# Five products of the folded gated weight as three fp32r matmuls on split operands

## The chip, the cores and the metric

The kernel runs on one core of a Trainium2 chip, in one launch. Its time is the device time of the whole program in microseconds (us), from repeated runs. The core has five engines that run side by side and wait for each other by semaphores: TensorE (PE in the profile; its weight loads are PEld), VectorE (DVE), ScalarE (ACT), GpSimd (POOL) and SyncE (SP), which here only issues DMAs. Matmul results land in PSUM, in banks of 128 x 512 fp32 values; everything else lies in SBUF.

## The reference

The program is three layers: a linear attention with a decaying state, a mixture of eight experts (one per token, with a skip test), and a gated layer. The change concerns the last one's weights only:

```python
def _attn_ref(r, k, v, w, u):            # per step t, for all batches and heads
    cur = einsum('bhd,bhe->bhde', u[None] * k[t], v[t])
    y[t] = einsum('bhd,bhde->bhe', r[t], state + cur)
    state = w[None, :, :, None] * state + einsum('bhd,bhe->bhde', k[t], v[t])

def _moe_ref(x, w_skip, w_gate, w1, w2): # N, D, E, F = 3072, 384, 8, 1024
    xc = x[x @ w_skip > 0]
    e_idx, probs = argmax(xc @ w_gate), softmax(xc @ w_gate)
    for e in range(E):
        y[mask] = gate_w[mask, None] * (maximum(xc[mask] @ w1[e], 0) @ w2[e])
    out[do_compute] = xc + y

def _moe2_ref(x, w1, w2, w3, w_out):     # w3: 1024 x 1024, w_out: 1024 x 384
    a = x @ w1
    b = x @ w2
    h = a * b @ w3
    return (h @ w_out)
```

All inputs are fp32. Since (a * b) @ w3 @ w_out is (a * b) @ (w3 @ w_out), the kernel computes the folded weight wf = w3 @ w_out (1024 x 384) once, from the weights, and the gated layer then has one matmul less.

## The kernel before, in words

The program has a block of stages and then the gated layers. In the block, each engine runs its part of the attention (`attention`), then of the routing (`routing`: which token goes to which expert, as lists of slots), then of the experts (`experts`: eight experts, one tile of up to 224 tokens each). The order on every engine is the order in which the code is written; nothing is rearranged. Engines move on independently, held only by the waits.

The fold is cut into eight chunks of 128 rows of w3, and its pieces are put between the other work by hand. For chunk i there are five steps, all methods of `Fold`:

- `load` (SP, L58 to L61) brings chunk i of w3 (512 KB) to SBUF; `load_w_out` brings w_out in two halves (768 KB each) once.
- `turn` (TensorE, L68 to L74) transposes the chunk in eight 128x128 pieces into two PSUM banks.
- `turned` (ACT, L76 to L81) copies the two banks to `w3T`, in two halves of 128x512.
- `product` (TensorE, L83 to L95) multiplies the eight slices of 128 rows with w_out into one bank, 384 columns: fp32 operands, one `matmul` call per slice, which is two instructions in the trace. It may be cut in quarters of two slices.
- `taken` (ACT, L97 to L101) copies the bank to `wf`.

`s_T`, `s_Tout`, `s_W` and `s_Wout` count these steps, and each waits for the one before by such a count. Product 0 and turns 0 and 1 stand at the end of the attention stage, turn 2 to the first half of product 5 in the routing, the second half of product 5 behind the transposes of the first expert's tokens, product 6 behind the experts and product 7 around the start of the gated layers.

Between the fold's pieces in the routing stand the routing's own matmuls: the counts (L832 to L839, into `p_count`), which wait for `s_m` from DVE and release the chain of short DVE operations behind `s_mm`; the transposes of the gate (L842 to L844); and the list matmuls (L848 to L855, into `p_list`), which wait for the one-hot tables (`s_token`, `s_near`) and release the two DVE operations that make `slot_token`. GpSimd gathers the first expert's tokens by that list (L1042), SP loads the first expert's weights w1 and w2 (1536 KB each), and ACT and DVE split w1 in a rounded part `hi` (fp32r) and the rest `lo` (`first_w1_hi`, `first_w1_lo`, L1034 and L1037).

The expert and gated layers already run with such splits: a product x y is computed as x_hi y_hi + x_hi y_lo + x_lo y_hi, three matmuls on fp32r operands (L1265, L1281, L1508, L1523).

Of the kernel before, what the change touches and what calls it, by code (L numbers as in the profile page):

```python
# [12 lines left out]
P = 128  # L13
# [20 lines left out]
LINE = 1024  # L34
# [4 lines left out]
class Fold:  # L39
# [3 lines left out]


    def __init__(self, nc, sb, sem, ident, s_ident, w3, w_out):
# [4 lines left out]
        self.w3T = [sb(f"w3T{i}", [P, self.KF, P]) for i in range(3)]  # L50
# [4 lines left out]
        self.s_T, self.s_Tout = sem("fold_T"), sem("fold_Tout")  # L55
# [58 lines left out]
def attention(nc, env, sem, r, k, v, w, u, xbuf):  # L114
# [16 lines left out]
    with ExitStack() as ctx:  # L131
# [311 lines left out]
        def _(act):  # L443
# [83 lines left out]
        def _(dve):  # L527
# [83 lines left out]
            schedule(dve, ((masks, 0), (states, -1), (bonuses, 1), (rT_out, 1), (x_out, -1), (k_decay, 2)), 2, 1, extra)  # L611
            dve.wait_ge(s_lg, 1)
# [114 lines left out]
def routing(nc, env, NT, E, NSL, CAP, ROOM, xbuf):  # L727
# [8 lines left out]
    with ExitStack() as ctx:  # L736
# [20 lines left out]
        pos = sb("pos", [P, E, NT])  # L757
        over = sb("over", [P, E, NT])
# [53 lines left out]
        def _(pool):  # L812
# [16 lines left out]
        def _(pe):  # L829
            fold.turn(pe, 2, p_T[0])  # L830
            fold.product(pe, 1, p_W[1], (0, 1, 2))
# [8 lines left out]
            fold.product(pe, 1, p_W[1], (3,))  # L840
# [7 lines left out]
            fold.product(pe, 3, p_W[1], (0, 1, 2))  # L848
# [7 lines left out]
            fold.product(pe, 3, p_W[1], (3,))  # L856
# [29 lines left out]
        def _(dve):  # L886
# [69 lines left out]
            ex.first_w1_lo(dve)  # L956
# [732 lines left out]
```

## Time and profile before

| | |
|---|---|
| median of 3 runs | 615.23 us (614.32, 615.23, 615.3) |
| profiled execution: span from first to last instruction | 612.5 us |
| TensorE busy | 595.1 us, 97% of the span, 7355 matmul instructions |
| DVE busy | 286.4 us, 47% |
| ACT busy | 228.1 us, 37% |
| GpSimd busy | 156.5 us, 26% |
| DMA | 67.80 MB, mean 111 GB/s |
| mean granted TensorE clock | 0.994 of full speed |

The page of the profile gives the span of the profiled execution and no other time of it; the median of the timed runs is 2.7 us above that span. Busy time counts an instruction from its start to its end; matmuls overlap each other, so the spacing of their starts, and not their mean duration, tells what one costs. Idle time in front of an instruction, in square brackets at the end of a timeline row, names what ended it.

### The profile page before, as it was taken

Reading aid. Unit: us, or ns where it says so; the run is one execution under the profiler, and the core shown is the slowest. Engines: PE = TensorE matmul, PEld = TensorE weight load, DVE = VectorE, ACT = ScalarE, POOL = GpSimd, SP = SyncE. Lnnn points to the kernel's source line nnn. Section 1 sums busy time; section 2 is a strip of 40 time slices with the busy share of each in tenths; the row PEclk is TensorE's granted clock in tenths of the full one; section 3 lists DMA queues with packets and bytes.
Section 4 is the critical chain, followed back from the end, with each engine's and each line's share of the span. In section 5 each row is a group of like instructions: output and inputs, shape, how many; then the busy total and the mean of one; then the engine's idle time right before and its main releaser. Section 6 shows DMA issues by size and latency. Waiting matters only on the chain.

```text
span 612.5 us, 17307 instructions
## 1 busy us (share of the span) xinstructions
PE 595.1 (97%) x7355; PEld 532.3 (87%) x7355; DVE 286.4 (47%) x459; ACT 228.1 (37%) x410; POOL 156.5 (26%) x179
## 2 busy tenths in 40 slices
PE   6699999999999999999999999999999999999997
PEld 6699999766999999999688888888898888888886
DVE  5489889283777777774121332232132133223212
ACT  3156666444665555552321222132132122213212
POOL 7568887215055544441230000000000000000000
PEclk9899999999999999999999999999999999999999
DMA  7779997596566777630400030020011001001001
GB/s 130 133 145 187 188 184 188 206 313 241 181 237 246 277 274 271 237 130 20 164 1 0 1 103 1 1 103 1 0 57 48 1 1 51 1 1 51 1 0 52
DMA packets 104258, 67.80 MB, mean 111 GB/s; under 512 B 79708, under 2 KB 98272, under 8 KB 104216
## 3 DMA queue, kind: packets, MB, share of 16 engines
q1 hardware_dynamic: 76360, 57.91, 30.8%
q10 hardware_dynamic: 25552, 4.72, 4.1%
q0 software_dynamic: 2304, 4.59, 2.3%
q8 instruction: 29, 0.48, 0.3%
q14 instruction: 13, 0.11, 0.1%
HBM read 55.92 MB, written 12.20 MB: 111 GB/s over the span
## 4 chain that ended last, share of the span: by engine, by line
PE 50%; DVE 0%; ACT 0%; issue 0%
PE gl_pab L1508 32%; PE gl_po L1523 8%; PE p_pair L1523 8%; PE gl_pab L1496 1%; PE p_pair L93 0%; DVE gl_g_lo L1590 0%; DVE gl_g_sb L1588 0%; ACT gl_g_hi L1568 0%; ACT gl_a_sb L1565 0%; DVE gl_o_sb L1601 0%
## 5 line engine op out<-in xcount | busy, mean ns | idle before, releaser
L1588 DVE TENSOR_TENSOR gl_g_sb<-gl_a_sb,gl_pab 128x512 f32<-128x512 f32 x48 | 33.0, 688 | 186.3 <-ACT gl_a_sb L1565 186.3
L1508 PE MATMUL gl_pab<-gl_xT_hi,wm_lo 128*128 128x512 f32 x288 | 112.9, 392 | 0.0
L1508 PE MATMUL gl_pab<-gl_xT_lo,wm_hi 128*128 128x512 f32 x288 | 112.8, 392 | 0.0
L1508 PE MATMUL gl_pab<-gl_xT_hi,wm_hi 128*128 128x512 f32 x288 | 112.1, 389 | 0.0
L1565 ACT ACTIVATE gl_a_sb<-gl_pab 128x512 f32<-128x512 f32 x48 | 28.8, 599 | 183.9 <-PE gl_pab L1508 183.9
L1508 PEld LDWEIGHTS gl_pab<-gl_xT_hi,wm_lo 128*128 128x128 f32 x288 | 54.0, 188 | 11.4
L1508 PEld LDWEIGHTS gl_pab<-gl_xT_hi,wm_hi 128*128 128x128 f32 x288 | 54.1, 188 | 10.6 <-DVE gl_xT_lo L1595 0.3
L1508 PEld LDWEIGHTS gl_pab<-gl_xT_lo,wm_hi 128*128 128x128 f32 x288 | 54.0, 188 | 10.5
L1265 PE MATMUL ex_ph<-ex_xT_hi,ew_w_hi 128*128 128x224 f32 x192 | 52.9, 275 | 0.0
L1265 PE MATMUL ex_ph<-ex_xT_hi,ew_w_lo 128*128 128x224 f32 x192 | 52.7, 274 | 0.0
L1265 PE MATMUL ex_ph<-ex_xT_lo,ew_w_hi 128*128 128x224 f32 x192 | 52.7, 274 | 0.0
L1590 DVE TENSOR_TENSOR gl_g_lo<-gl_g_sb,gl_g_hi 128x512 fp32r<-128x512 f32 x48 | 33.2, 692 | 33.5 <-ACT gl_g_hi L1568 33.5
L1568 ACT ACTIVATE gl_g_hi<-gl_g_sb 128x512 fp32r<-128x512 f32 x48 | 30.3, 632 | 36.2 <-DVE gl_g_sb L1588 36.2
L1281 PE MATMUL p_pair<-ew_w_hi,ex_h_hi 128*96 128x384 f32 (+1 forms) x128 | 43.4, 339 | 0.0
L1281 PE MATMUL p_pair<-ew_w_hi,ex_h_lo 128*96 128x384 f32 (+1 forms) x128 | 43.0, 336 | 0.0
L1281 PE MATMUL p_pair<-ew_w_lo,ex_h_hi 128*96 128x384 f32 (+1 forms) x128 | 43.0, 336 | 0.0
L1042 POOL DMA_INDIRECT ew_x_in<-xbuf,slot_token x16 | 22.5, 1406 | 71.3 <-DVE ex_x_new L1392 50.3
L93 PE MATMUL p_pair<-wo,w3T 128*128 128x384 f32 x112 | 38.8, 489 | 0.5 <-PEq L1652 0.4
L1265 PEld LDWEIGHTS ex_ph<-ex_xT_hi,ew_w_hi 128*128 128x128 f32 x192 | 36.8, 192 | 0.2
L1265 PEld LDWEIGHTS ex_ph<-ex_xT_lo,ew_w_hi 128*128 128x128 f32 x192 | 36.8, 192 | 0.1
L1265 PEld LDWEIGHTS ex_ph<-ex_xT_hi,ew_w_lo 128*128 128x128 f32 x192 | 36.9, 192 | 0.0
L1523 PE MATMUL gl_po<-gl_wf_hi,gl_g_hi 128*128 128x384 f32 x96 | 33.5, 349 | 0.7 <-DVE gl_g_lo L1590 0.7
(197 smaller groups left out, 1223.3 us busy)
## 6 DMA issues: line engine op xcount, KB each, us to landing
w_in<-in_moe_w SPq DMA_DIRECT2D x8, 1536.0 KB
ew_w_in<-in_moe_w SPq DMA_DIRECT2D x8, 1536.0 KB
w_in<-in_moe_w SPq DMA_DIRECT2D x14, 512.0 KB, 9.4
k_in<-in_k SPq DMA_DIRECT2D x48, 96.0 KB
v_in<-in_v ACTq DMA_DIRECT2D x48, 96.0 KB, 3.5
r_in<-in_r SPq DMA_DIRECT2D x48, 96.0 KB
w_in<-xbuf SPq DMA_DIRECT2D x12, 384.0 KB, 4.1
out<-gl_o_sb SPq DMA_DIRECT2D x12, 384.0 KB, 2.4
```

The source lines that it names most:

```text
L93: m = pe.matmul(bank[:, 0:self.DM], self.w3T[i % 3][:, g, :], self.wo[:, g, :], start=(g == 0), stop=(g == self.KF - 1), skip_group_check= ...
L1042: pool.indirect_dma_start(self.x_in[slot][0:tokens.shape[0], i, :], None, xbuf[:, :], bass.IndirectOffsetOnAxis(ap=tokens, axis=0), bounds ...
L1265: m = pe.matmul(p_h[g][:, f % 2, 0:width(t)], a[:, k, cols], b[:, k, 0:width(t)], start=(k == 0 and n == 0), stop=(k == KD - 1 and n == 2))
L1281: m = pe.matmul(p_y[i][0:n_tok, 0:DM], a[:, f, cols], b[:, f, :], start=(f == 0 and n == 0), stop=(f == KF - 1 and n == 2))
L1496: m = pe.transpose(p_ab[part][k % 2][:, i * P:(i + 1) * P], x_in[t.slot][:, i, k * P:(k + 1) * P], ident[:, :])
L1508: m = pe.matmul(p_ab[f % 2][w][:, :], a[:, w * KD + k, cols], b[t.slot][:, k, :], start=(k == 0 and n == 0), stop=(k == KD - 1 and n == 2))
L1523: m = pe.matmul(p_o[i][:, 0:DM], a[f % 2][:, cols], b[:, f, :], start=(f == 0 and n == 0), stop=(f == KF - 1 and n == 2))
L1565: act.activation(a_sb[f % 2][:, :], p_ab[f % 2][0][:, :], ACT.Copy).then_inc(s_a, 1)
L1568: act.activation(g_hi[f % 2][:, :], g_sb[f % 2][:, :], ACT.Copy).then_inc(s_ghi, 1)
L1588: dve.tensor_tensor(g_sb[f % 2][:, :], a_sb[f % 2][:, :], p_ab[f % 2][1][:, :], ALU.mult).then_inc(s_g, 1)
L1590: dve.tensor_tensor(g_lo[f % 2][:, :], g_sb[f % 2][:, :], g_hi[f % 2][:, :], ALU.subtract).then_inc(s_glo, 1)
```

## The change

Products 1 to 5 no longer run on fp32 operands. w_out is split once into `wo_hi` and `wo_lo` (ACT converts, DVE subtracts, four quarters each). The transposes of chunks 1 to 5 are converted to fp32r by ACT (`hi`, two buffers) and the rest is subtracted into `lo` (two buffers): for chunks 1, 4 and 5 by DVE straight from PSUM (`rest_dve`), for chunks 2 and 3 by GpSimd, for which ACT also makes a plain fp32 copy (`rest_pool`). Each slice is then three matmuls on fp32r operands. Products 0, 6 and 7 stay fp32. The fourth quarters of products 1 and 3, which stood behind the counts and behind the list, now stand ahead of them with the rest. `pos` and `over` share the memory of `key` and `dif`; `wo_hi` and `wo_lo` lie where the experts' `w2_hi` and `w2_lo` lie later, and ACT's first write there waits for product 5.

```diff
-
-    def __init__(self, nc, sb, sem, ident, s_ident, w3, w_out):
+    RAW = {0: 0, 2: 1, 3: 0, 6: 0, 7: 1}
+    BY_POOL = (2, 3)
+    BY_DVE = (1, 4, 5)
...
-        self.w3T = [sb(f"w3T{i}", [P, self.KF, P]) for i in range(3)]
+        self.w3T = [sb(f"w3T{i}", [P, self.KF, P]) for i in range(2)]
+        shape = [P, self.KF, P]
+        self.hi = [sb("w3T_hi0", shape, F32R), at("w3T_hi1", shape, F32R, top - 3 * 4 * FM)]
+        self.lo = [at(f"w3T_lo{i}", shape, F32R, top - (2 - i) * 4 * FM) for i in range(2)]
...
+    def out_hi(self, act, q):
+
+        rows = slice(2 * q, 2 * q + 2)
+        act.wait_ge(self.s_wo[q // 2], 16)
+        act.activation(flat(self.wo_hi[:, rows, :]), flat(self.wo[:, rows, :]), ACT.Copy).then_inc(self.s_wohi, 1)
+
+    def out_lo(self, dve, q):
+        rows = slice(2 * q, 2 * q + 2)
+        dve.wait_ge(self.s_wohi, q + 1)
+        dve.tensor_tensor(flat(self.wo_lo[:, rows, :]), flat(self.wo[:, rows, :]), flat(self.wo_hi[:, rows, :]), ALU.subtract).then_inc(self.s_wolo, 1)
+
     def turn(self, pe, i, banks):
         wait(pe, self.s_w3[i % 3], 16 * (i // 3 + 1))
         wait(pe, self.s_Tout, 2 * i)
+        if i in (4, 5):
+            wait(pe, self.s_raw, 2 * (i - 3))
+        if i in (2, 6, 7):
+            wait(pe, self.s_dlo, {2: 2, 6: 4, 7: 6}[i])
         for g in range(self.KF):
             m = pe.transpose(banks[g // 4][:, (g % 4) * P:(g % 4 + 1) * P], self.w3_in[i % 3][:, g * P:(g + 1) * P], self.ident[:, :])
         m.then_inc(self.s_T, 1)
...
     def turned(self, act, i, banks):
         wait(act, self.s_T, i + 1)
-        wait(act, self.s_W, i - 2)
+        if i in (0, 6, 7):
+            wait(act, self.s_plo, {0: 0, 6: 4, 7: 2}[i])
+            for h in range(2):
+                act.activation(self.half(self.w3T[self.RAW[i]], h), banks[h][:, :], ACT.Copy).then_inc(self.s_Tout, 1)
+            return
+        wait(act, self.s_W, i - 1 if i > 2 else 0)
         for h in range(2):
-            act.activation(flat(self.w3T[i % 3][:, 4 * h:4 * h + 4, :]), banks[h][:, :], ACT.Copy).then_inc(self.s_Tout, 1)
+            act.activation(self.half(self.hi[i % 2], h), banks[h][:, :], ACT.Copy).then_inc(self.s_Tout, 1)
+        if i in self.BY_POOL:
+            for h in range(2):
+                act.activation(self.half(self.w3T[self.RAW[i]], h), banks[h][:, :], ACT.Copy).then_inc(self.s_raw, 1)
+
+    def rest_dve(self, dve, i, banks):
+
+        for h in range(2):
+            dve.wait_ge(self.s_Tout, 2 * i + h + 1)
+            dve.tensor_tensor(self.half(self.lo[i % 2], h), banks[h][:, :], self.half(self.hi[i % 2], h), ALU.subtract).then_inc(self.s_dlo, 1)
+
+    def rest_pool(self, pool, i):
+
+        for h in range(2):
+            pool.wait_ge(self.s_raw, 2 * (i - 2) + h + 1)
+            pool.tensor_tensor(self.half(self.lo[i % 2], h), self.half(self.w3T[self.RAW[i]], h), self.half(self.hi[i % 2], h), ALU.subtract).then_inc(self.s_plo, 1)
...
         if 0 in quarters:
-            wait(pe, self.s_Tout, 2 * i + 2)
             wait(pe, self.s_Wout, i - 1)
         n = self.KF // 4
         for q in quarters:
+            h = q // 2
+            if q % 2 == 0:
+                wait(pe, self.s_Tout, 2 * i + h + 1)
+                if i in self.BY_POOL:
+                    wait(pe, self.s_plo, 2 * (i - 2) + h + 1)
+                if i in self.BY_DVE:
+                    wait(pe, self.s_dlo, 2 * self.BY_DVE.index(i) + h + 1)
+            if i == 1:
+                pe.wait_ge(self.s_wolo, q + 1)
             for g in range(q * n, (q + 1) * n):
                 if i == 0 and g % (self.KF // 2) == 0:
                     pe.wait_ge(self.s_wo[g // (self.KF // 2)], 16)
-                m = pe.matmul(bank[:, 0:self.DM], self.w3T[i % 3][:, g, :], self.wo[:, g, :],
-                              start=(g == 0), stop=(g == self.KF - 1), skip_group_check=True)
+                if i in (0, 6, 7):
+                    m = pe.matmul(bank[:, 0:self.DM], self.w3T[self.RAW[i]][:, g, :], self.wo[:, g, :],
+                                  start=(g == 0), stop=(g == self.KF - 1), skip_group_check=True)
+                    continue
+                hi, lo = self.hi[i % 2], self.lo[i % 2]
+                for n3, (a, b) in enumerate(((hi, self.wo_hi), (hi, self.wo_lo), (lo, self.wo_hi))):
+                    m = pe.matmul(bank[:, 0:self.DM], a[:, g, :], b[:, g, :],
+                                  start=(g == 0 and n3 == 0), stop=(g == self.KF - 1 and n3 == 2), skip_group_check=True)
         if 3 in quarters:
             m.then_inc(self.s_W, 1)
...
                 if f is y_out and at(c, j, NT - 1):
                     fold.turned(act, 0, [p_AU[:, i, :] for i in range(2)])
+                if f is y_out and at(c, j, NT):
+                    for q in range(3):
+                        fold.out_hi(act, q)
                 if f is y_out and at(c, j, NT + 2):
                     fold.turned(act, 1, [p_R[:, i, :] for i in range(2)])
+                    fold.out_hi(act, 3)
                     act.wait_ge(s_Y, BASE + NT + 1)
...
             schedule(dve, ((masks, 0), (states, -1), (bonuses, 1), (rT_out, 1), (x_out, -1), (k_decay, 2)), 2, 1, extra)
+            for q in range(3):
+                fold.out_lo(dve, q)
+            fold.rest_dve(dve, 1, [p_R[:, i, :] for i in range(2)])
+            fold.out_lo(dve, 3)
             dve.wait_ge(s_lg, 1)
...
+        pos, over = key, dif
...
                 pool.memset(x[:, :], 0.0).then_inc(s_clear, 1)
+            for i in fold.BY_POOL:
+                fold.rest_pool(pool, i)
...
             fold.turn(pe, 2, p_T[0])
-            fold.product(pe, 1, p_W[1], (0, 1, 2))
+            fold.product(pe, 1, p_W[1])
             pe.wait_ge(s_m, 2)
...
             pe.matmul(p_tot, tb.ones[:, :], last[1], start=False, stop=True, skip_group_check=True).then_inc(s_mm, 1)
-            fold.product(pe, 1, p_W[1], (3,))
             fold.turn(pe, 3, p_T[1])
             pe.wait_ge(s_gate, 1)
...
             fold.product(pe, 2, p_W[0])
             fold.turn(pe, 4, p_T[0])
-            fold.product(pe, 3, p_W[1], (0, 1, 2))
+            fold.product(pe, 3, p_W[1])
             pe.wait_ge(s_near, 1)
...
             m.then_inc(s_list, 1)
-            fold.product(pe, 3, p_W[1], (3,))
             fold.turn(pe, 5, p_T[1])
             fold.product(pe, 4, p_W[0], (0, 1))
...
             dve.sem_inc(env["s_listed"], 1)
-            ex.first_w1_lo(dve)
+            fold.rest_dve(dve, 4, p_T[0])
+            ex.first_w1_lo(dve, (0, 1))
+            fold.rest_dve(dve, 5, p_T[1])
+            ex.first_w1_lo(dve, (2, 3))
...
+        self.w2_hi, self.w2_lo = sb("w2_hi", [P, KF, DM], F32R), sb("w2_lo", [P, KF, DM], F32R)
...
             def w2_part(t, g):
+                if g == 0 and is_first(t):
+                    act.wait_ge(fold.s_W, 6)
                 if g == 0:
...
+        behind = nc.sbuf_base + 5 * 4 * KD * FM
+        env["fold"].wo_hi, env["fold"].wo_lo = (at(n, [P, FM // P, DM], F32R, behind + i * 4 * DM * FM // P) for i, n in enumerate(("wo_hi", "wo_lo")))
```

On TensorE, around product 1 and the counts in the routing stage, this is the order before (`w_in` are the buffers of w3's chunks, `ro_pT` the banks of the transposes, `p_pair` those of the products):

```order
L73 MATMUL ro_pT<-ident,w_in 128x128 x8
L93 MATMUL p_pair<-wo,w3T 128x384 x6
L834 MATMUL ro_p_count<-tb_mine,tb_before 128x192
...
L839 MATMUL ro_p_count<-ro_earlier,tb_ones 128x8
L93 MATMUL p_pair<-wo,w3T 128x384 x2
L73 MATMUL ro_pT<-ident,w_in 128x128 x8
```

and after the change, where of the 24 matmuls of product 1 the first three and the last stand:

```order
L96 MATMUL ro_pT<-ident,w_in 128x128 x8
L153 MATMUL p_pair<-wo_hi,w3T_hi_49 128x384
L153 MATMUL p_pair<-wo_lo,w3T_hi_49 128x384
L153 MATMUL p_pair<-wo_hi,w3T_lo_51 128x384
...
L153 MATMUL p_pair<-wo_hi,w3T_lo_51 128x384
L903 MATMUL ro_p_count<-tb_mine,tb_before 128x192
...
L908 MATMUL ro_p_count<-ro_earlier,tb_ones 128x8
L96 MATMUL ro_pT<-ident,w_in 128x128 x8
```

Product 1 stood in two pieces around the counts, six slices and two; it now stands whole ahead of them. Product 3 and the list matmuls are the same case.

On DVE, behind the list matmuls of the routing stage, this is the order before, with the semaphores that each waits for (`ro_list` is counted up by the list matmuls, `ew_w1hi` by ACT's split of w1):

```order
L952 COPY ro_lst<-ro_p_list 128x40 [waits ro_list]
L953 SCALAR_TENSOR_TENSOR slot_token<-ro_p_list,ro_lst 128x40 [waits ro_d]
L1037 TENSOR_TENSOR ew_w_lo<-w_in,ew_w_hi 128x3x256 [waits ro_table,ew_w1hi]
L1037 TENSOR_TENSOR ew_w_lo<-w_in,ew_w_hi 128x3x256 [waits ew_w1hi] x3
L958 TENSOR_SCALAR n_over<-ro_ends 128x1
```

and after:

```order
L1019 COPY ro_lst<-ro_p_list 128x40 [waits ro_list]
L1020 SCALAR_TENSOR_TENSOR slot_token<-ro_p_list,ro_lst 128x40 [waits ro_d]
L121 TENSOR_TENSOR w3T_lo_50<-ro_pT,w3T_hi 128x512 [waits ro_table,fold_Tout]
L121 TENSOR_TENSOR w3T_lo_50<-ro_pT,w3T_hi 128x512 [waits fold_Tout]
L1107 TENSOR_TENSOR ew_w_lo<-w_in,ew_w_hi 128x3x256 [waits ew_w1hi] x2
L121 TENSOR_TENSOR w3T_lo_51<-ro_pT,w3T_hi_49 128x512 [waits fold_Tout] x2
L1107 TENSOR_TENSOR ew_w_lo<-w_in,ew_w_hi 128x3x256 [waits ew_w1hi] x2
L1028 TENSOR_SCALAR n_over<-ro_ends 128x1
```

The subtractions for product 4 (`w3T_lo_50`) stand directly behind the list, those for product 5 (`w3T_lo_51`) between the two pairs of w1's splits.

## Rows read from the trace of the kernel before

**Rows 1.** The page's slices of TensorE's busy time, in tenths, 40 equal slices.

```profile
PE   6699999999999999999999999999999999999997
```

**Rows 2.** Stage: us; PE, PEld, DVE, ACT, POOL busy (instructions); clock, DMA share, GB/s.

```profile
122.00:156.00 34.00, 34.00 (x173) 22.63 (x172) 19.42 (x41) 15.04 (x28) 10.14 (x13) 1.00 0.83 282
```

**Rows 3.** Timeline of TensorE, routing stage: start, us, engine, line, operation.

```profile
121.40 1.09 PE L73 MATMUL ro_pT<-ident,w_in 128*128 128x128 f32 x8
122.33 4.04 PE L93 MATMUL p_pair<-wo,w3T 128*128 128x384 f32 x12
126.20 0.25 PE L834 MATMUL ro_p_count<-tb_mine,tb_before 128*128 128x192 bf16 x1
...
128.25 1.04 PE L73 MATMUL ro_pT<-ident,w_in 128*128 128x128 f32 x8
...
129.34 5.33 PE L93 MATMUL p_pair<-wo,w3T 128*128 128x384 f32 x16
134.50 1.04 PE L73 MATMUL ro_pT<-ident,w_in 128*128 128x128 f32 x8
...
139.25 1.02 PE L853 MATMUL ro_p_list<-ro_vals,ro_oh_lo 128*128 128x80 bf16 x24
140.11 1.53 PE L93 MATMUL p_pair<-wo,w3T 128*128 128x384 f32 x4
...
148.39 1.04 PE L73 MATMUL ro_pT<-ident,w_in 128*128 128x128 f32 x8
...
154.75 0.56 PE L1265 MATMUL ex_ph<-ex_xT_hi,ew_w_hi 128*128 128x224 f32 x1
```

**Rows 4.** Timeline of TensorE, an expert's second matmul: two starts, 22 intervals apart.

```profile
219.01 0.34 PE L1281 MATMUL p_pair<-ew_w_lo,ex_h_hi 128*96 128x384 f32 x1
...
222.83 0.34 PE L1281 MATMUL p_pair<-ew_w_hi,ex_h_lo 128*96 128x384 f32 x1
```

**Rows 5.** Timeline of ACT: fold copies, and the split of the first expert's w1.

```profile
118.11 1.08 ACT L81 ACTIVATE w3T<-p_R 128x512 f32<-128x512 f32 x2
...
124.14 1.07 ACT L81 ACTIVATE w3T<-ro_pT 128x512 f32<-128x512 f32 x2
...
137.75 3.04 ACT L1034 ACTIVATE ew_w_hi<-w_in 128x768 fp32r<-128x768 f32 x4 [1.09 <-DMA w_in<-in_moe_w]
```

**Rows 6.** DVE: timeline of the routing stage, then a group of 90 to 112 us.

```profile
121.80 0.56 DVE L614 TENSOR_TENSOR lg<-lg_parts 128x216 f32<-128x216 f32 x1 [7.92 <-ACT lg_parts L507]
...
133.84 3.43 DVE L948 TENSOR_TENSOR ro_oh_lo<-tb_col,ro_lo 128x1536 bf16<-128x1536 bf16 x2
...
140.89 3.58 DVE L1037 TENSOR_TENSOR ew_w_lo<-w_in,ew_w_hi 128x768 fp32r<-128x768 f32 x4
...
L563 DVE TENSOR_TENSOR A_m<-p_pair,causal 128x512 f32<-128x512 f32 x3 | 2.1, 692 | 1.1 <-PE p_pair L405 1.1
```

**Rows 7.** SP's issues of w3's chunks, and chunk 5's time from issue to landing.

```profile
128.52 1.92 SPq L61 DMA_DIRECT2D w_in<-in_moe_w  x1
...
w_in<-in_moe_w SPq DMA_DIRECT2D x1, 512.0 KB, 10.5
...
137.42 0.37 SPq L61 DMA_DIRECT2D w_in<-in_moe_w  x1
```

**Rows 8.** DMA: one stretch by stage; hardware queue, 144.5:145 and 145:145.5.

```profile
134.00:135.00 1.00, 1.00 (x8) 0.69 (x7) 1.00 (x1) 0.29 (x1) 0.00 (x0) 1.00 1.01 385
...
q1 hardware_dynamic: 17, 0.06, 30.0%
...
q1 hardware_dynamic: 6, 0.01, 6.3%
```

**Rows 9.** GpSimd's two-input operation and first gather; the stretch of low clock.

```profile
L653 POOL TENSOR_TENSOR rk<-r_in,k_in 128x384 f32<-128x384 f32 x4 | 4.0, 1009 | 2.8 <-DVE k_dec L599 2.8
...
141.74 1.27 POOL L1042 DMA_INDIRECT ew_x_in<-xbuf,slot_token  x1 [17.53 <-DVE slot_token L953]
...
17.00:21.00 4.00, 4.00 (x163) 3.81 (x161) 1.50 (x3) 0.62 (x2) 3.84 (x5) 0.65 0.89 168
```

More of the change, by code:

```diff
@@ L39, with __init__ @@
 class Fold:
-    def __init__(self, nc, sb, sem, ident, s_ident, w3, w_out):
+    RAW = {0: 0, 2: 1, 3: 0, 6: 0, 7: 1}
+    BY_POOL = (2, 3)
+    BY_DVE = (1, 4, 5)
+    def __init__(self, nc, sb, sem, at, top, ident, s_ident, w3, w_out):
         FM, DM = w_out.shape
@@ L54, in __init__ @@
         self.s_wo = [sem(f"fold_wo{i}") for i in range(2)]
-        self.s_T, self.s_Tout = sem("fold_T"), sem("fold_Tout")
+        self.s_T, self.s_Tout, self.s_raw = sem("fold_T"), sem("fold_Tout"), sem("fold_raw")
+        self.s_dlo, self.s_plo = sem("fold_dlo"), sem("fold_plo")
+        self.s_wohi, self.s_wolo = sem("fold_wohi"), sem("fold_wolo")
         self.s_W, self.s_Wout = sem("fold_W"), sem("fold_Wout")
@@ L74, in turn, with half @@
         m.then_inc(self.s_T, 1)
+    def half(self, x, h):
+        return flat(x[:, 4 * h:4 * h + 4, :])
     def turned(self, act, i, banks):
         wait(act, self.s_T, i + 1)
-        wait(act, self.s_W, i - 2)
-        for h in range(2):
-            act.activation(flat(self.w3T[i % 3][:, 4 * h:4 * h + 4, :]), banks[h][:, :], ACT.Copy).then_inc(self.s_Tout, 1)
+        if i in (0, 6, 7):
[4 more added lines that the diff above has]
+        wait(act, self.s_W, i - 1 if i > 2 else 0)
+        for h in range(2):
+            act.activation(self.half(self.hi[i % 2], h), banks[h][:, :], ACT.Copy).then_inc(self.s_Tout, 1)
[10 more added lines that the diff above has]
+            pool.tensor_tensor(self.half(self.lo[i % 2], h), self.half(self.w3T[self.RAW[i]], h), self.half(self.hi[i % 2], h), ALU.subtract).then_inc(self.s_plo, 1)
     def product(self, pe, i, bank, quarters=(0, 1, 2, 3)):
         if 0 in quarters:
-            wait(pe, self.s_Tout, 2 * i + 2)
             wait(pe, self.s_Wout, i - 1)
@@ L756, in routing @@
         earlier = sb("earlier", [P, E * NT], BF16)
-        pos = sb("pos", [P, E, NT])
-        over = sb("over", [P, E, NT])
+        pos, over = key, dif
         is_over = sb("is_over", [P, E, NO])
@@ L1010, in __init__ @@
         self.w1, self.w2, self.NG = w1, w2, KF // 2
+        self.w2_hi, self.w2_lo = sb("w2_hi", [P, KF, DM], F32R), sb("w2_lo", [P, KF, DM], F32R)
         self.w1_in, self.w2_in = w1_in, sb("w2_in", [P, KF, DM])
         self.w1_hi, self.w1_lo = sb("w1_hi", [P, KD, FM], F32R), sb("w1_lo", [P, KD, FM], F32R)
-        self.w2_hi, self.w2_lo = sb("w2_hi", [P, KF, DM], F32R), sb("w2_lo", [P, KF, DM], F32R)
         self.x_in = [sb(f"x_in{i}", [P, 2, DM]) for i in range(2)]
@@ L1060, in first_w1_hi, with first_w1_lo @@
             self.split_w1_hi(act, g)
-    def first_w1_lo(self, dve):
-        for g in range(self.NG):
+    def first_w1_lo(self, dve, parts):
+        for g in parts:
             dve.wait_ge(self.s_w1hi, g + 1)
@@ L1625, in program, with at @@
         s_iota = sem("s_iota")
+        def at(n, s, d, offset):
+            return nc.alloc_sbuf_tensor_at(n, s, d, offset=offset)
         ident = sb("ident", [P, P])
@@ L1632, in program @@
             "w_gate": moe_w_gate, "w_skip": moe_w_skip, "wm": (moe2_w1, moe2_w2),
-            "fold": Fold(nc, sb, sem, ident, s_iota, moe2_w3, moe2_w_out),
+            "fold": Fold(nc, sb, sem, at, nc.sbuf_usable_end // LINE * LINE, ident, s_iota, moe2_w3, moe2_w_out),
             "s_wmlo": sem("s_wmlo"), "lg": sb("lg", [P, E + 1, N // P]), "seq": S,
```

## The prediction

> **What bounds the kernel now.** I read the page's 40 slices first: TensorE is busy for nine tenths or more in all but the first two and the last [rows 1]. The stage table then gives the stretch with the change: between 122 and 156 us TensorE is busy for 34.00 of 34.00 us, at a granted clock of 1.00, which is 2.4 GHz [rows 2]. So what TensorE is given less to do there moves everything behind it forward, up to the point where something else is not ready. That is why the timelines of the same 34 us come next: TensorE's own, then ACT, DVE, the loads and GpSimd.
>
> The profiled span is 612.5 us, the median of the three runs 615.23. The page gives no other time of the profiled execution; the 2.7 us around the span are taken to stay, and what I work out in the span is taken off the median.
>
> **What goes and what comes on TensorE.** An fp32 product of 8 slices is 16 matmul instructions in the trace. Product 2 starts at 129.34 and turn 4 behind it at 134.50: 5.16 us [rows 3]. Three fp32r matmuls a slice make 24 of the same 128x384 shape. The expert stage runs that shape: from the one at 219.01 to the one at 222.83 lie 22 intervals, 3.82 us, 0.174 us each [rows 4]. 24 of them are 4.17 us, so a product loses 0.99 us and five lose 4.9 us. Break-even would be 5.16 / 24 = 0.215 us an instruction. All five products lie in the stretch where TensorE never idles, so 4.9 us is the most that the change can bring.
>
> The Trainium skill, in TensorE: Matmul & The Clock Gate (Back-to-back issue gap), puts the isolated spacing at full clock at columns over 2.4 GHz and a fixed 2.5 ns: 162.5 ns for 384 columns. By that the five products would lose 6.3 us. The trace's 174 ns, with a weight load for every matmul, decides here against the rule.
>
> **Where TensorE then has to wait.** I walk its order with the durations of [rows 3]. Turn 2 ends at 122.33. Before it stands a new wait, for the two subtractions that read product 1's transposes out of the PSUM banks. ACT writes hi 1 at 118.11 to 119.19 as it wrote w3T [rows 5]; DVE sat idle for 7.92 us up to 121.80, it is free from 113.9 on, and an operation on 128x512 from PSUM is 0.69 us [rows 6]; the four splits of w_out on DVE, 0.9 us each, fit beside them; so they are done at about 120.1, and turn 2 started at 121.40. Nothing is lost. The four conversions of w_out on ACT are 128x768, of which the four at 137.75 took 3.04 us [rows 5]; three stand ahead of the 118.11 conversion and one behind it, at about 120.0, before TensorE's logits are there.
>
> Product 1 is now whole: 122.33 to 126.50. The counting matmuls that the routing chain on DVE waits for, at 126.20 before, come 0.3 us later. This chain ends in the one-hot table at 133.84 + 3.43 = 137.27 [rows 6]; I carry the 0.3 us as an upper bound, 137.6. The counts take 0.7 us (126.20 to 128.25 less a quarter of a product, 1.29), turn 3 and the gate's transposes 1.09 (128.25 to 129.34): 128.3. Product 2 needs lo 0 from GpSimd: ACT starts on turn 2's transposes at 124.14 [rows 5], at 0.54 us a half for hi and then for the raw copy, so the raw halves are ready at 125.8 and 126.3, and a GpSimd product of 128x384 takes 1.01 us [rows 9], so 1.35 for 512 columns by the same rate; if it were twice that, the second half would be ready at 131.2 and would cost 0.8 us. I take no wait, since 1.35 is worked out from the same two-input operation. Product 2: 132.5.
>
> Turn 4 needs chunk 4 of w3. No row gives its landing. It stands in the queue directly ahead of the first expert's w1 (1536 KB), which ACT was waiting for until 137.75 [rows 5]. At 385 GB/s [rows 8] that is 4.1 us: chunk 4 at 133.7; and it was there at 134.50, when turn 4 started without idle time. From below, 132.5, if w1's packets were already mixed with it. I take 133.3: a wait of 0.8 us, between 0 and 1.5. A turn takes 0.9 us (121.40 to 122.33), product 3 4.17, the list's 24 matmuls 0.86 (139.25 to 140.11 before): product 3 ends at 138.4, later than the one-hot table, so no wait for that; the list matmuls are issued until 139.25. Chunk 5 lands at 128.52 + 10.5 = 139.0 [rows 7], just in time. Turn 5 until 140.1.
>
> Product 4 now waits for DVE, which subtracts lo only behind the list. Before, the last list matmul ended at 139.25 + 1.02 = 140.27 [rows 3], and DVE, with the two short operations that make the list, went on to the next at 140.89 [rows 6]. So 139.4 + 0.6 = 140.0, first half of lo at 140.7: TensorE waits 0.6 us. Behind it in DVE's queue are the splits of w1, 0.9 us each; with four lo halves between them the last ends at about 146.4; it is wanted at about 151, no cost. Half of product 4, 2.09: 142.8. Turn 6 needs ACT's conversion of product 5's transposes. ACT splits w1 from 137.75 to 140.79 [rows 5], then takes product 3 and converts until 142.3: no wait, with 0.5 us to spare. If chunk 4 came at once this spare is used up, so it is no extra gain. Turn 6 0.9, half a product 2.09: 145.8.
>
> Turn 7 needs chunk 7. SP issued it at 137.42 [rows 7], held up by a full queue and not by TensorE, so the change doesn't bring it forward. The hardware queue still moved 17 packets between 144.5 and 145 and 6 between 145 and 145.5 [rows 8]: it lands about 145.5. So TensorE comes just behind it; turn 7 starts at 145.8, against 148.39 [rows 3]: 2.6 us earlier. Behind turn 7 stands all of product 5, worth another 0.99. The token gather ahead of the first expert was issued at 141.74 on GpSimd [rows 9] and comes 0.9 us earlier with the list; its transposes would be at 148.7. No cost.
>
> **Sum:** 4.95 us of matmuls, less 0.8 (chunk 4) and 0.6 (lo for product 4), is 3.6 us. 615.23 - 3.6 = 611.6 us. Behind the first expert every load and gather is released by work that moves with TensorE, so I carry the whole gain to the end: the slices up to the last but one leave under a tenth of TensorE idle each [rows 1]. The new wait of ACT before the first expert's w2 asks for product 5, which ACT has then already copied out. The own range: chunk 4 anywhere from 132.5 to 134.0 and chunk 7 from 145.2 to 146.2 give gains of 2.9 to 4.0, 611.2 to 612.3.
>
> **The rivals.**
> A, the loads come early enough and DVE's half wait is covered: only matmul time counts, gain 4.2 to 4.9, 610.3 to 611.0. For it: the packets thin out at 145, and lo's first half is only 0.69 us. Against it: chunk 7 at 145.5 alone caps the gain at 148.39 - 145.5 + 1.0 = 3.9. It would need chunk 7 by 144.9. 0.17.
>
> B, the loads bind harder. The gather starts 0.9 us earlier, at a time when the engines are still moving 17 packets of the hardware queue in half a us [rows 8], and pushes chunk 7 back; each us of that is a us of gain lost. With chunk 7 at 146.5 to 147.7 the gain is 1.7 to 2.9, 612.3 to 613.5. Against it: the gather only swaps places with bytes that had to go anyway. 0.21.
>
> C, split matmuls cost more than in the expert stage, since ACT, DVE, GpSimd and the loads all read and write SBUF here: at 0.20 us an instruction a product gains 0.36, the sum 1.8 less what waits remain; at 0.215 nothing. With the waits the kernel stands within 0.2% of now. For it: no split product of this kind runs in this stretch. Against it: the same shape keeps 0.174 us at 219 us with DVE and ACT at work. 0.09.
>
> D, slower: the clock falls. In this kernel the granted clock was 0.65 between 17 and 21 us although TensorE was busy for all 4.00 of these us; 4 us at 0.65 cost 1.4 us [rows 9]; in the slice of 15.3 us before and around it TensorE had been busy for six tenths [rows 1]. Between 122 and 152 us it now gets up to three gaps of under 1 us. One such fall would cost 1.4 us and leave 2.2 of gain; the kernel becomes slower than before from three falls on, 4.2 us, and over the 0.2% bound from four, about 617.2. The Trainium skill, in TensorE: Matmul & The Clock Gate (HAM oscillation), tells of a kernel whose waits between bursts of matmuls bring the clock down each time; by this rule gaps as short as these would be harmless, but no run here shows it yet. 0.03.
>
> **The numbers.** The forecast itself 0.50, A 0.17, B 0.21, C 0.09, D 0.03. What can be told from no change is 0.2%, 1.2 us: under 614.0 is faster, over 616.5 slower. B and A are faster as is the forecast; B's far end and C fall within. Faster 0.86, same 0.11, slower 0.03. The range for 8 in 10 takes in A's upper half and B nearly whole: 610.5 to 613.5.
>
> **What the profile after would show.** The matmuls of products 1 to 5 at a spacing of 0.174 us; turn 2 with no wait; a wait before turn 4 of 0 to 1.5 us that ends with a load; one of about 0.6 us before product 4 that ends with DVE's lo; turn 7 at 145.5 to 146; the first expert matmul, 154.75 before [rows 3], at about 151.1; the same distance from there to the end. I am wrong if product 4 does not wait or waits for over 1 us, if turn 7 starts later than 146.5, or if the 3.6 us that the first expert matmul has gained are not there at 290 us.

## The result, and the profile after

| | before | after |
|---|---|---|
| median of the comparison | 615.30 us (614.32 to 617.04, 7 runs) | 612.32 us (611.74 to 613.36, 7 runs) |
| profiled execution: span | 612.5 us | 610.8 us |

The ratio is 0.995, with a 95% interval of 0.9936 to 0.9963: faster by 3.0 us, with an interval of 2.3 to 3.9. Run once more beside the experiments, the changed kernel had 612.59 us (612.25 to 613.96, 5 runs) against 614.80 (13 runs) before, 0.9964 [0.995, 0.9977]: 2.2 us, interval 1.4 to 3.1. The changed kernel's profiled execution took 612.74 us, 1.9 above its span, where 2.7 were taken for before.

TensorE starts the routing at another moment in every execution, since the attention ahead of it varies: turn 2 stands between 120.91 and 123.34 us in the profiled executions of all these kernels, before and changed alike. So all times below are counted from the start of turn 2 (121.40 before [rows 3], 121.93 after), unless they are a row's own.

The timeline of TensorE after (start, duration, engine, line, operation, in brackets the idle time and what ended it), the rows that answer to [rows 3]; of product 1 the first four matmuls:

```profile
121.93 1.09 PE L96 MATMUL ro_pT<-ident,w_in 128*128 128x128 f32 x8
122.78 0.42 PE L153 MATMUL p_pair<-wo_hi,w3T_hi 128*128 128x384 f32 x1
123.04 0.34 PE L153 MATMUL p_pair<-wo_lo,w3T_hi 128*128 128x384 f32 x1
123.21 0.34 PE L153 MATMUL p_pair<-wo_hi,w3T_lo 128*128 128x384 f32 x1
123.39 0.34 PE L153 MATMUL p_pair<-wo_hi,w3T_hi 128*128 128x384 f32 x1
...
127.03 0.26 PE L903 MATMUL ro_p_count<-tb_mine,tb_before 128*128 128x192 bf16 x1
...
132.87 0.34 PE L153 MATMUL p_pair<-wo_hi,w3T_lo 128*128 128x384 f32 x1
134.85 1.09 PE L96 MATMUL ro_pT<-ident,w_in 128*128 128x128 f32 x8 [1.64 <-DMA w_in<-in_moe_w]
...
139.99 1.04 PE L921 MATMUL ro_p_list<-ro_vals,ro_oh_lo 128*128 128x80 bf16 x24
140.85 1.07 PE L96 MATMUL ro_pT<-ident,w_in 128*128 128x128 f32 x8
142.47 0.41 PE L153 MATMUL p_pair<-wo_hi,w3T_hi 128*128 128x384 f32 x1 [0.55 <-DVE w3T_lo L121]
...
147.59 1.03 PE L96 MATMUL ro_pT<-ident,w_in 128*128 128x128 f32 x8
...
153.29 0.26 PE L1335 MATMUL ex_ph<-ex_xT_hi,ew_w_hi 128*128 128x224 f32 x1
```

Turn 2 has no wait, the matmuls follow each other every 0.174 us, and there are two waits: 1.64 us for chunk 4 (134.85) and 0.55 us for DVE (142.47). The first expert matmul stands 31.36 us behind turn 2, against 33.35 before. Before, its row was 0.56 us long, since it still stood behind the product; by the rows' ends the gain is 2.3 us: 155.31 - 121.40 = 33.91, and 153.55 - 121.93 = 31.62.

The stretches of the kernel after (us, then busy time of PE, PEld, DVE, ACT, POOL; clock, DMA share, GB/s), the first of them answering to [rows 2]:

```profile
122.00:152.00 30.00, 27.81 (x201) 26.58 (x201) 22.77 (x44) 16.03 (x31) 13.14 (x15) 1.00 0.81 271
152.00:286.00 134.00, 134.00 (x996) 131.64 (x995) 97.56 (x129) 74.22 (x114) 59.02 (x41) 1.00 0.60 215
```

TensorE was never idle in the stage before; now 2.19 of 30 us are idle. Behind it TensorE is busy for all of the next 134 us, and nothing is given back: from the end of that first expert row to the end of the span it is 457.2 us before (612.5 - 155.31) and 457.25 after (610.8 - 153.55). The span itself gained only 1.7, because the attention ended 0.5 us later in this execution.

The timelines of DVE and GpSimd in the same stage show what the prediction did not weigh: GpSimd's subtractions overlap DVE's chain of short operations. Before, DVE:

```profile
130.39 0.18 DVE L937 SCALAR_TENSOR_TENSOR ro_dest_i<-ro_closed,ro_dest 128x24 int32<-128x24 f32 x1
130.61 0.18 DVE L938 TENSOR_SCALAR ro_hi_i<-ro_dest_i 128x24 int32<-128x24 int32 x1
```

After, DVE:

```profile
131.24 0.58 DVE L1004 SCALAR_TENSOR_TENSOR ro_dest_i<-ro_closed,ro_dest 128x24 int32<-128x24 f32 x1
131.85 1.21 DVE L1005 TENSOR_SCALAR ro_hi_i<-ro_dest_i 128x24 int32<-128x24 int32 x1
...
136.11 3.43 DVE L1015 TENSOR_TENSOR ro_oh_lo<-tb_col,ro_lo 128x1536 bf16<-128x1536 bf16 x2
```

And GpSimd:

```profile
126.32 2.51 POOL L127 TENSOR_TENSOR w3T_lo<-w3T,w3T_hi 128x512 fp32r<-128x512 f32 x2 [1.58 <-ACT w3T L115]
130.48 2.54 POOL L127 TENSOR_TENSOR w3T_lo<-w3T,w3T_hi 128x512 fp32r<-128x512 f32 x2 [1.66 <-ACT w3T L115]
```

GpSimd subtracts chunk 3's rest from 130.48 to 133.02. In that time two DVE operations on 24 elements take 0.58 and 1.21 us instead of 0.18 each, and the second ends at 133.06, with GpSimd's. That is 1.43 us on the chain to the one-hot table. The one-hot table ends at 136.11 + 3.43 = 139.54, 17.61 behind turn 2, where it was 15.87 before [rows 6]: 1.74 later, of which 0.30 is the later counts. The run without GpSimd's subtractions (e2, below) tests this reading. TensorE reaches the list at 139.99, so in this kernel chunk 4's wait hides it, with 0.45 us to spare.

### The profile page after: what moved, and what is told of

It reads as the page before. It is cut to its first block, busy times and chain, and to the rows that moved or that the text cites. A ratio compares the mean times of both kernels' runs of the same rounds, so it can differ in the third digit from the quotient of the medians.

```text
span 610.8 us, 17417 instructions
## 1 busy us (share of the span) xinstructions
PE 592.7 (97%) x7395; PEld 539.9 (88%) x7395; DVE 294.9 (48%) x469; ACT 232.7 (38%) x418; POOL 163.7 (27%) x183
## 4 chain that ended last, share of the span: by engine, by line
PE 50%; DVE 0%; ACT 0%; issue 0%
PE gl_pab L1580 32%; PE gl_po L1595 8%; PE p_pair L1595 8%; PE gl_pab L1568 1%; PE p_pair L148 0%; DVE gl_g_lo L1662 0%; DVE gl_g_sb L1660 0%; ACT gl_g_hi L1640 0%; ACT gl_a_sb L1637 0%; DVE gl_o_sb L1673 0%
## 5 line engine op out<-in xcount | busy, mean ns | idle before, releaser
L1399 ACT ACTIVATE ew_w_hi<-ew_w_in 128x768 fp32r<-128x768 f32 x32 | 26.9, 841 | 18.1 <-PE p_pair L1351 18.1
```

The costliest lines, as they stand in the source:

```text
L1399: act.activation(flat(w2_hi[:, 2 * g:2 * g + 2, :]), flat(w2_in[:, 2 * g:2 * g + 2, :]), ACT.Copy).then_inc(s_w2hi, 1)
```

## The experiments

In e2 and e3 the rest (`lo`) of chunks 2 and 3 is a plain copy, so products 2 and 3 come out wrong there; the other kernels compute what the changed kernel does. The distance is the time in us from the start of turn 2 to the first expert matmul, in the one profiled execution of each kernel; positions are in us behind the start of turn 2. The kernel before was run beside each group: 614.61 us (17 runs) for e1 to e4, 614.88 (29) for e5, e6, e8 and e9, 614.80 (13) for e10 to e12 and r1.

**e1, chunk 4 first.** The load of chunk 4 goes ahead of the last stores of x.

```diff
-            fold.load(sp, [3])
+            fold.load(sp, [3, 4])
...
-            fold.load(sp, [4])
```

> The changed kernel, with the load of chunk 4 issued directly behind chunk 3, ahead of the last 1.5 MB of stores of x, in place of behind them. In the changed kernel TensorE waits 1.64 us before turn 4 for this load. Theory 1 (the loads alone bind): this wait goes and all of it is gained, until chunk 7 binds turn 7; from turn 2 to the first expert matmul the distance falls from 31.36 to 29.8 us, the kernel gains 1.5 us on the changed one, 610.8 us. Theory 2 (DVE's routing chain has become late, its one-hot table is ready 17.6 us behind turn 2's start, because GpSimd's subtractions hold up short DVE operations): turn 4 starts 1.6 us earlier, but the list matmuls then wait about 1.2 us for the table, which showed only 0.45 us before them; the distance falls by 0.4 us to 30.9, 611.9 us.

Measured: 612.12 us (610.25 to 613.34, 6 runs), 0.9944 [0.9928, 0.9961]. TensorE's waits between turn 2 and the experts (us in total, times, longest):

```profile
PE ro_p_list L920 <- DVE ro_oh_lo L1014: 0.9, 1, 0.9
PE p_pair L153 <- DVE w3T_lo L121: 0.6, 1, 0.6
```

The load's wait is gone and the table's has come up, as theory 2 had it: the list's first half is issued at 16.16, the second waits 0.89 for DVE (about 1.2 expected). The first expert matmul stands at 30.53 instead of 31.36. So the load cost 1.8 us, and with it gone only 0.8 of that is gained; the rest is lost again to the table. The medians can't tell this kernel from the changed one; the distances differ by 0.8, in one execution each.

**e2, the same without GpSimd's subtraction.** ACT's raw copy goes straight into `lo`.

```diff
-            wait(act, self.s_plo, {0: 0, 6: 4, 7: 2}[i])
+            wait(act, self.s_raw, {0: 0, 6: 4, 7: 2}[i])
...
-                act.activation(self.half(self.w3T[self.RAW[i]], h), banks[h][:, :], ACT.Copy).then_inc(self.s_raw, 1)
+                act.activation(self.half(self.lo[i % 2], h), banks[h][:, :], ACT.Copy).then_inc(self.s_raw, 1)
...
-            for i in fold.BY_POOL:
-                fold.rest_pool(pool, i)
```

> The same with GpSimd's four subtractions left out: ACT writes a plain copy of the transposes to lo for chunks 2 and 3, so products 2 and 3 get a wrong lo, at the same cost on ACT and TensorE. Theory 1: no difference from the run with chunk 4 first, 610.8 us both. Theory 2: the short DVE operations that took 0.58 and 1.21 us beside GpSimd's subtraction of chunk 3 are back at 0.18 each, the table is ready at 15.9 us behind turn 2, the list matmuls don't wait, and the distance to the first expert matmul is 29.8 us, 1.1 us shorter than with chunk 4 first alone: about 610.8 us against 611.9.

Measured: 612.53 us (611.66 to 613.4, 6 runs), 0.9957 [0.9942, 0.9972]; distance 31.92. DVE's timeline, the rows that answer to those above, and TensorE's waits:

```profile
130.62 0.18 DVE L1001 SCALAR_TENSOR_TENSOR ro_dest_i<-ro_closed,ro_dest 128x24 int32<-128x24 f32 x1
130.84 0.18 DVE L1002 TENSOR_SCALAR ro_hi_i<-ro_dest_i 128x24 int32<-128x24 int32 x1
...
134.07 3.43 DVE L1012 TENSOR_TENSOR ro_oh_lo<-tb_col,ro_lo 128x1536 bf16<-128x1536 bf16 x2
```

```profile
PE ro_pT L96 <- DMA w_in<-in_moe_w: 2.5, 2, 1.6
```

Without GpSimd's subtractions the two short operations are back at 0.18 us each and the table is ready at 16.00 (134.07 + 3.43 - 121.50), 1.6 earlier than in the changed kernel. That part of theory 2 is shown. Its gain is not: the list no longer waits, nor does product 4, but turn 5 waits 1.59 us for chunk 5 and turn 7 0.93 us for chunk 7, which neither theory had. With the table's wait gone TensorE runs into the next load. e1's table wait covers only a part of this: it put turn 5 at 18.09, without it turn 5 would be due at 17.03, and here it starts at 18.79. Chunk 5 itself came 1.0 us later than in e1 (issued at 5.18 and 13.6 us to landing, against 5.29 and 12.5), with the loads issued in the same order.

**e3, only GpSimd's subtraction gone**, with the loads as in the changed kernel (e2's edit without e1's).

> The changed kernel with only GpSimd's four subtractions left out (lo of chunks 2 and 3 is a plain copy made by ACT), chunk 4's load where it was. Both theories: TensorE still waits 1.6 us before turn 4, and this wait covers DVE's delay, so the time is that of the changed kernel, 612.3 us, within 0.3. Theory 2 adds: the one-hot table comes 1.5 to 1.7 us earlier all the same. If the time falls by over 0.6 us, GpSimd's work delays something else that I have not seen.

Measured: 612.22 us (610.86 to 615.73, 7 runs), 0.995 [0.9936, 0.9965]: the changed kernel's time. The two short operations take 0.18 us each, and the table is ready at 15.99, 1.6 us earlier, as expected. While chunk 4 is late, the subtraction costs nothing that the median can tell. The profiled execution was its longest, 615.73 us, with a distance of 33.68. Its stretches:

```profile
133.00:136.20 3.20, 0.81 (x5) 0.49 (x3) 2.98 (x5) 1.48 (x2) 0.00 (x0) 1.00 0.97 355
...
138.53:142.53 4.00, 4.00 (x18) 4.00 (x17) 0.00 (x0) 2.66 (x4) 0.00 (x0) 0.71 1.04 399
```

Chunk 4 came late enough for a wait of 2.40 us, TensorE was busy for 0.81 of 3.20 us, and then the granted clock fell. Two matmuls of its timeline in that time:

```profile
138.16 0.52 PE L153 MATMUL p_pair<-wo_lo,w3T_hi 128*128 128x384 f32 x1
138.48 0.52 PE L153 MATMUL p_pair<-wo_hi,w3T_lo 128*128 128x384 f32 x1
```

The spacing was 0.32 us there, that of the 1.2 GHz level, for ten matmuls: 1.5 us more. With chunk 4 later by 0.8 us this makes up the 2.3 us by which the distance exceeds the changed kernel's. It is what rival D described, once, at a cost near the 1.4 us that it was given, though behind a longer gap than D's of under 1 us. That the wait brought the fall about is likely from the order of the two, and not shown by this one execution.

**e4, the order alone.** On the kernel before: products 1 and 3, still fp32, stand whole ahead of the counts and the list.

```diff
-            fold.product(pe, 1, p_W[1], (0, 1, 2))
+            fold.product(pe, 1, p_W[1])
...
-            fold.product(pe, 1, p_W[1], (3,))
```

> The kernel before, with only the order of the change: products 1 and 3 stay fp32 but stand whole ahead of the counts and of the list. The counts come 1.3 us later (a quarter product, 1.29 us), so does DVE's chain: table at 138.5 in before's times against 137.27. Product 3 ends at 140.5, so the list doesn't wait for it. The list itself and the token gather come 1.3 us later than before, lists' consumers at 141.6 and later; the gather lands 2 us before its transposes. Time as before, 615.3, within 0.3 us. A rival: the late list delays the gather beyond the transposes of the first expert's tokens at 151.8, up to 1 us slower.

Measured: 614.95 us (613.76 to 616.53, 10 runs), 1.0002 [0.999, 1.0015]; distance 33.25, TensorE with no wait. The counts stand at 6.09, the split product brings them to 5.10: 0.99 us for one product, by itself. The order alone costs and gains nothing, as expected.

**e8, the order undone.** The changed kernel with the last quarters of products 1 and 3 back behind the counts and the list.

> The changed kernel with only the order undone: the last quarter of product 1 stands behind the counts and that of product 3 behind the list again, as before. The list matmuls are reached 1.04 us earlier, 17.0 us behind turn 2, and the second half of the token table is ready at 17.1 (counts 0.3 us earlier than in the changed kernel): at most 0.2 us of wait. The list is made 0.9 us earlier, so lo for product 4 is made 0.9 us earlier and its wait of 0.55 us goes: distance 30.8 us, 0.5 us faster than the changed kernel. The rival, by which the list must stand behind product 3 because the table is late: a wait of over 0.6 us before the list, and no gain or a loss.

Measured: 613.15 us (611.65 to 613.6, 6 runs), 0.9962 [0.9948, 0.9976]; distance 31.48 (31.36 after). TensorE now waits 0.41 us for DVE ahead of the counts, 0.62 for chunk 4 and 0.99 for the table, and not for product 4's rest, since a quarter of product 3 covers that. So the 0.5 us that were expected did not come; the rival that was named did, a wait of over 0.6 us before the list and no gain. The order moves the waits; it is worth nothing that these runs can tell.

**e5, e6 and e9, GpSimd moved away from the short operations.** Its two subtractions of chunk 3 are held until DVE has made `ro_oh_hi` and, for the second, `ro_lo`: e6 does that alone, e5 with chunk 4 first, e9 also with the first expert's w2 loaded behind chunk 7.

```diff
-    def rest_pool(self, pool, i):
+    def rest_pool(self, pool, i, gates):
...
+            if i == 3:
+                pool.wait_ge(gates[h], 1)
...
+            dve.sem_inc(s_lo, 1)
```

> Chunk 4's load behind chunk 3's, as in the first run, and GpSimd's two subtractions of chunk 3 moved in time and nothing left out: the first waits until DVE has made the one-hot table of slots, the second until DVE has converted the low bits. Theory 2 of the first runs (GpSimd's instruction holds up the short DVE operations that overlap it): the two that took 0.58 and 1.21 us are at 0.18 again, the token table is ready at about 16.2 us behind turn 2 against 17.6, and the list matmuls don't wait. What binds then is the loads, as in the run without GpSimd: turn 5 waits for chunk 5 until 17.8 to 18.8, turn 7 for chunk 7 until 25 to 26. Distance turn 2 to first expert matmul 30.2 to 31.9, time as the changed kernel's within 0.6 us. The rival (it was GpSimd's late table that cost most of the forecast gain): 29.8 us, 1.5 us faster than the changed kernel.

> The same, and the load of the first expert's w2 (1.5 MB) issued behind chunk 7 in place of ahead of it. w2 is wanted only when ACT splits it, 32 us behind turn 2. If the queue of loads is what binds turn 7, chunk 7 lands about 3.8 us earlier and turn 7 no longer waits; only turn 5's wait for chunk 5 (0.5 to 1.6 us) and the 0.6 us for lo before product 4 stay: distance 29.6 to 30.6 us, 0.8 to 1.8 us faster than the changed kernel, 610.3 to 611.4. If the loads bind nothing any more, no difference to the run before it in this list.

> The changed kernel with only GpSimd's subtractions of chunk 3 moved in time, chunk 4's load where it was. The short DVE operations are at 0.18 us, the token table 1.3 us earlier, but TensorE's wait for chunk 4 (1.6 us) stands before it, so time and distance (31.4 us) are those of the changed kernel, within 0.4 us.

Measured: e5 614.28 us (612.79 to 615.71, 12 runs), 0.9989 [0.9979, 1.0]; e9 613.79 (613.09 to 614.95, 12 runs), 0.998 [0.9971, 0.9989]; e6 613.84 (613.1 to 615.74, 10 runs), 0.9986 [0.9975, 0.9997]. By their medians all three are slower than the changed kernel, and they miss what was expected; the intervals lie above the changed kernel's 0.9936 to 0.9963, but those of e6 and e9 overlap the one of its second run (0.995 to 0.9977). The timelines of e5, DVE first:

```profile
131.09 0.18 DVE L1006 TENSOR_SCALAR ro_hi_i<-ro_dest_i 128x24 int32<-128x24 int32 x1
...
133.90 1.24 DVE L1012 TENSOR_SCALAR ro_lo_i<-ro_dest_i 128x24 int32<-128x24 int32 x1
...
135.50 4.50 DVE L1017 TENSOR_TENSOR ro_oh_lo<-tb_col,ro_lo 128x1536 bf16<-128x1536 bf16 x2
```

GpSimd and TensorE:

```profile
132.87 2.23 POOL L129 TENSOR_TENSOR w3T_lo<-w3T,w3T_hi 128x512 fp32r<-128x512 f32 x1 [4.42 <-DVEq L1010]
135.55 2.83 POOL L129 TENSOR_TENSOR w3T_lo<-w3T,w3T_hi 128x512 fp32r<-128x512 f32 x1 [0.45 <-DVEq L1014]
```

```profile
135.25 0.41 PE L155 MATMUL p_pair<-wo_hi,w3T_hi 128*128 128x384 f32 x1 [1.53 <-ACT w3T_hi L112]
...
138.53 0.41 PE L155 MATMUL p_pair<-wo_hi,w3T_hi 128*128 128x384 f32 x1 [0.93 <-POOL w3T_lo L129]
```

The short operations are back at 0.18 us with the subtraction moved, as they were with it left out. But the conflict has only moved: GpSimd's subtraction, 1.26 us by itself (2.51 for two), takes 2.23 and 2.83 beside the two-input operations on the tables, the next short one takes 1.24, and the table 4.50 instead of 3.43. Product 3 needs the results at once: TensorE waits 1.53 and 0.93 us. Its first wait is put down to ACT's conversion, which happened to end at about that time, but that one is of turn 4 and for product 4; what product 3 asked for was GpSimd's first half, which ended at 132.87 + 2.23 = 135.10. Both waits are for GpSimd. The distance is 32.43, 1.9 more than in e1; in e6 it is 32.47 and in e9 32.49. The three have their loads in three different orders, so it is the moved subtraction, and not a load, that sets the stretch.

**e10, e11, e12, the loads.** e10: chunk 4 first as in e1, and the first expert's w2 behind chunk 7; e12: w2 alone; e11: e10 with product 3 in fp32, so that GpSimd has chunk 2 only. r1 is the changed kernel again.

```diff
-            fold.load(sp, [3])
+            fold.load(sp, [3, 4])
...
-            fold.load(sp, [4])
...
-            ex.load_w2(sp, 0)
...
+            ex.load_w2(sp, 0)
```

> The changed kernel with two loads moved and nothing else: chunk 4 behind chunk 3, ahead of the stores of x, and w2 of the first expert behind chunk 7. Theory (loads and the late table bind in turn): no wait before turn 4 and turn 7 in any execution, the list's second half still waits 0.9 us for the table, product 4 still 0.55 us for lo: distance 30.5 us, 0.8 us faster than the changed kernel. The rival (GpSimd's and DVE's shared work alone sets the stretch, the loads cost nothing): the time of the changed kernel.

> The same two loads moved, and product 3 back on fp32, so that GpSimd has no subtraction beside the making of the token table (four products split, not five). Product 3 costs 5.16 us again in place of 4.17, the table is ready at about 16 us behind turn 2, the list is reached at 17.1 and doesn't wait. If the fifth split product only trades matmul time for the wait for the table, the distance is 30.3 to 30.6 us, the same as with five products split and the same loads moved, within 0.2% in time. If the wait for the table were cheap, this kernel would be 1 us slower than that one.

> The changed kernel with only w2's load moved behind chunk 7. In the changed kernel's profiled execution turn 7 did not wait for chunk 7; chunk 4's wait of 1.64 us stands before it. So no gain: distance 31.4, time as the changed kernel's within 0.4 us. If chunk 7 binds in other executions, 0.3 to 0.8 us faster.

> The changed kernel once more, beside the three others of this list, on the same chip: distance from turn 2 to the first expert matmul 31.4 us within 0.5 (chunk 4's landing differs from one execution to the next), time 0.3 to 0.5% below the kernel before.

| | median (runs) | ratio to before [95%] | first expert matmul |
|---|---|---|---|
| r1 | 612.59 us (5) | 0.9964 [0.995, 0.9977] | 31.68 |
| e12 | 612.19 us (8) | 0.9956 [0.9941, 0.9971] | 31.23 |
| e11 | 612.47 us (5) | 0.9954 [0.9941, 0.9968] | 30.45 |
| e10 | 611.04 us (6) | 0.9939 [0.9925, 0.9954] | 30.57 |

e10 has the lowest median of all kernels run, 3.8 us below before and 1.55 below the changed kernel beside it (r1); the two intervals just overlap, so that second difference is likely but not certain. Its distance is e1's to 0.04 us (30.53), so w2's place brings nothing within the stage. The move does what it was meant to do: in e12 chunk 7 lands at 20.2 (issued at 135.33, 6.3 us to landing), in the changed kernel at 24.7 (137.89, 8.7 us). But there turn 7 stood at 25.66 and was not waiting for it. What is left in it, by TensorE's waits (the second is put down to ACT, but it is the wait of product 4 for DVE's rest, as in e1):

```profile
PE ro_p_list L919 <- DVE ro_oh_lo L1013: 0.9, 1, 0.9
PE p_pair L153 <- ACT wf L161: 0.6, 1, 0.6
```

e11 exchanges the table's wait for one split product less, and comes out level in the distance, as expected (30.45): what splitting product 3 gains on TensorE is lost again by having its rest made on GpSimd. The medians differ by 1.4 us, with intervals that overlap.

## Why the prediction was right, and where its sizes were off

**The matmuls.** Right. 24 matmuls at 0.174 us, so rival C's dearer matmuls did not come; with the same order before and after, product 1 alone is 0.99 us (e4 against after). 4.95 us for five was the term.

**Turn 2, product 2 and turn 6** do not wait, as worked out; GpSimd's two halves of chunk 2 took 2.51 us, 1.26 each, against 1.35 estimated.

**The wait for chunk 4** is the term that was mis-sized: 0.8 us forecast, within 0 to 1.5, and the row says 1.64, just outside. From the start that TensorE would have had (the last matmul of product 2 at 132.87, and 0.17) to 134.85 it is even 1.8, since an idle time counts only from the modelled end of the matmul before. Chunk 4 arrived 12.9 behind turn 2, 134.3 on the clock of before; the prediction's latest was 134.0. It had been placed by dividing the bytes behind it by the peak rate of one stretch [rows 8], as if w1's packets came strictly after it. And it is no fixed number: with the same loads ahead of it, and issued at the same 2.1 behind turn 2, chunk 4 let turn 4 start at 12.92, 13.27 (r1), 13.68 (e3), 12.78 (e12), 11.97 (e6) and 12.53 (e8), for waits of 1.64, 1.99, 2.40, 1.50, 0.69 and 0.62; in e8 TensorE itself came 0.6 later. With its load ahead of the stores the wait was 0 in all six kernels (e1, e2, e5, e9, e10, e11).

**The wait for product 4's rest** was forecast at 0.6 and is 0.55 by its row, 0.8 by the shift (turn 5 starts at 140.85 and takes 0.8; 142.47).

**Sum.** 4.95 - 1.8 - 0.8 = 2.35 us; measured 2.3 between turn 2 and the experts, 3.6 forecast. The median's 3.0 is nearer to the forecast than the stage's 2.3, and only by the spread of the runs: its interval begins at 2.3, and the second comparison has 2.2. That part of the agreement is luck. Turn 7 stood at 25.66, 147.1 on the clock of before: past the 146.5 that was given as the mark of a wrong step. The step that failed is that of chunk 4. The time, 612.32 us, stands where the forecast's own range and rival B's meet (612.3), the stage's 2.3 us in the middle of B's gain of 1.7 to 2.9, and by B's kind of mechanism, a load that binds harder. But B put it on chunk 7 pushed by an earlier gather, while here turn 7 did not wait, and the gather (142.48) came 20.55 behind turn 2, no earlier than before (20.34). Chunk 7 landed at 24.7, 146.1 on the clock of before and 0.6 later than forecast; TensorE came later still, which hid it.

**The table.** "No wait for that" came true for a reason that was not given, which is luck. The prediction carried 0.3 us onto the table; it was 1.74, because it took DVE's chain as independent of GpSimd's new work (e2 and e3 show that it was not). The chunk's wait hid it, and e1 brought it out. Had chunk 4 come as forecast, at 11.9, the list's second half would have been reached at about 17.5 and have waited some 0.2 us for the table at 17.6, an estimate from the rows of the changed kernel. The forecast 3.6 was not to be had in this order of work: e1 and e10, with no wait for loads at all, stand 0.8 us ahead of the changed kernel, which makes 3.1.

On such an overlap the Trainium skill, in SBUF — State Buffer (Who interferes with whom), says that VectorE and GpSimd share one pair of ports, held for a whole instruction, that VectorE instructions with two inputs in SBUF contend with GpSimd's reads, and that `tensor_scalar` may too. The traces agree: 0.58 and 1.21 us against 0.18, the second ending within 0.04 us of GpSimd's instruction, 2.23 and 2.83 against 1.26, 4.50 against 3.43.

**Carried to the end.** Right: 457.2 us before and 457.25 after.

**What stays open.** Why chunk 4's landing varies by 1.7 us between executions with the same issues ahead of it, and why chunks 5 and 7 came later in e2 than in e1. Whether e10's median gain over e1 (1.1 us, at an equal distance) is more than chance: the two were run at different times, and by their ratios to the kernel before, 0.9939 and 0.9944, it is 0.3 us.

## What to carry to other kernels

When an engine that never idles gets less to do, work out the supply of every step behind it, and expect several waits in a row: taking away the first (e1) or the second (e2) only shows the next. A load's landing is a spread, not a number; issue what the shortened engine needs ahead of stores that nobody waits for (here this took away a wait of 0.6 to 2.4 us, of which 0.8 us was kept in the distance). And work given to an idle GpSimd is not free for a chain of short VectorE operations, and moving it by a few us may only put it beside costlier ones.

## What was not expected of the hardware

A VectorE operation on 24 elements, 0.18 us, took up to 1.24 us beside a GpSimd subtraction of 128x512; and GpSimd's own took 2.83 instead of 1.26 beside VectorE's bf16 table. A single wait of TensorE of 2.40 us was followed by about 3.2 us of matmuls at half the clock in one execution (e3), whereas waits of 1.64 us (after) and 1.99 us (r1) were followed by none, at a granted clock of 1.00 in the whole stretch.
